# A chunked recurrence with two pairs of heads side by side: one row half per head, next inputs and last states in the gaps

## The reference

```python
for t in range(S):
    cur = einsum('bhd,bhe->bhde', u * k[t], v[t])
    y[t] = einsum('bhd,bhde->bhe', r[t], state + cur)
    state = w[t][..., None] * state + einsum('bhd,bhe->bhde', k[t], v[t])
```

## Time and profile before

| | us |
|---|---|
| median of 3 runs | 654.47 (654.16 to 656.38) |
| span of the profiled execution (first to last instruction) | 648.8 |
| of it: up to the first level of round 0 | 20.4 |
| round 0 | 28.3 |
| rounds 1 to 7 | 291.9 |
| last states, outputs, transposes of X | 21.1 |
| mixture up to its last stage | 55.6 |
| last stage | 231.5 |

### The profile page before, as it was taken

The page is one execution under the profiler, slowest core; times in us unless marked ns, Lnnn a source line. Parts: engine busy times, 40 slices in busy tenths (PEclk is TensorE's granted clock), DMA queues, the critical chain, the costliest instruction groups (busy, mean ns, idle before and its releaser), DMA issues.

```text
span 648.8 us, 20419 instructions
## 1 busy us (share of the span) xinstructions
PE 519.0 (80%) x8010; PEld 445.8 (69%) x8010; DVE 436.0 (67%) x968; ACT 397.5 (61%) x753; POOL 64.7 (10%) x79
## 2 busy tenths in 40 slices
PE   3756766877668668766686798699999999999996
PEld 2544655756457447564576434399999999999996
DVE  5668999898688688896797441465555555555553
ACT  3648686885576477865765313466566666656563
POOL 4011213112031031130310000000000000000000
PEclk9869898987698699886887899899999999999999
DMA  9995354362154143630057699311010101101010
GB/s 140 303 314 98 62 96 68 73 109 54 24 109 78 30 83 76 108 60 17 3 113 257 225 387 364 141 52 37 2 37 1 38 1 36 37 0 36 1 37 36
DMA packets 143325, 60.75 MB, mean 94 GB/s; under 512 B 126496, under 2 KB 139808, under 8 KB 142880
## 3 DMA queue, kind: packets, MB, share of 16 engines
q1 hardware_dynamic: 141264, 51.97, 33.9%
q10 hardware_dynamic: 2000, 7.86, 3.2%
HBM read 55.10 MB, written 4.72 MB: 92 GB/s over the span
## 4 chain that ended last, share of the span: by engine, by line
PE 63%; issue 13%; DVE 11%; ACT 10%; ACTq 1%; DVEq 1%; DMA 0%; SPq 0%
PE bank L708 11%; PE bank L710 10%; PE bank L709 10%; PE lbank L497 7%; ACT rkw L756 6%; PE tbank L449 4%; PE ybank L523 4%; PE bank L698 3%; DVE wprod L992 3%; DVE a_pack L1046 2%; PE tbank L459 2%; DVE rkw L1012 2%; PE bank L647 2%; PE bank L624 2%; PE bank L561 1%
## 5 line engine op out<-in xcount | busy, mean ns | idle before, releaser
L708 PE MATMUL bank<-wo_high,h_high 128*128 128x384 f32 x384 | 129.6, 337 | 1.8 <-DVE h_low L1212 1.6
L709 PE MATMUL bank<-wo_low,h_high 128*128 128x384 f32 x384 | 128.9, 336 | 0.0
L710 PE MATMUL bank<-wo_high,h_low 128*128 128x384 f32 x384 | 128.9, 336 | 0.0
L497 PE MATMUL lbank<-rhat,rkw 128*32 128x64 f32 x3456 | 81.5, 244 | 53.9 <-DVE a_pack L1046 36.8
L791 ACT ACTIVATE rhat<-rkw 48x384 f32<-48x384 f32 x160 | 85.0, 531 | 59.5 <-PE lbank L497 42.2
L497 PEld LDWEIGHTS lbank<-rhat,rkw 128*32 128x32 f32 x3456 | 69.9, 126 | 63.7 <-issue 61.9
L1210 DVE CAST h_high<-h_sq 128x384 fp32r<-128x384 f32 x128 | 46.0, 360 | 96.7 <-PE bank L710 87.9
L907 ACT ACTIVATE h_relu<-bank 128x384 f32<-128x384 f32 x128 | 62.9, 492 | 74.4 <-PE bank L698 74.1
L756 ACT ACTIVATE rkw<-tbank 128x384 f32<-128x384 f32 x96 | 74.4, 876 | 20.5 <-PE tbank L449 20.5
L449 PE MATMUL tbank<-ident,nat 128*128 128x128 f32 x288 | 62.7, 358 | 29.7 <-ACT rkw L756 16.7
L708 PEld LDWEIGHTS bank<-wo_high,h_high 128*128 128x128 f32 x384 | 72.6, 189 | 3.2 <-issue 2.8
(11 more groups left out here) (129 smaller groups left out, 639.2 us busy)
## 6 DMA issues: line engine op xcount, KB each, us to landing
w_sb<-in_moe_w_dram ACTq DMA_DIRECT2D x5, 1536.0 KB, 15.7
w_hi<-in_moe_w_dram SPq DMA_DIRECT2D x16, 384.0 KB, 8.1
nat<-in_r_dram SPq DMA_DIRECT2D x32, 144.0 KB, 3.2
nat<-in_k_dram SPq DMA_DIRECT2D x32, 144.0 KB, 3.8
nat<-in_w_dram SPq DMA_DIRECT2D x32, 144.0 KB, 3.9
mov<-in_v_dram SPq DMA_DIRECT2D x32, 144.0 KB, 3.3
v_tok<-in_v_dram SPq DMA_DIRECT2D x32, 144.0 KB, 3.3
w_sb<-in_moe_w_dram SPq DMA_DIRECT2D x3, 1536.0 KB, 7.4
```

Source lines behind the costliest of these rows:

```text
L497: last = nc.tensor.matmul(dst.rearrange("p (h t) -> p h t", h=2), kk[:, t0:t0 + SUB], rhat[s][:, :, tt:tt + SUB], start=True, stop=True)
L708: nc.tensor.matmul(acc, hi, wo_high[:, fb, :], start=(fb == 0), stop=False)
L709: nc.tensor.matmul(acc, hi, wo_low[:, fb, :], start=False, stop=False)
L710: last = nc.tensor.matmul(acc, lo, wo_high[:, fb, :], start=False, stop=(fb == NF - 1))
```

## The change

Four things change in the recurrence, and a few small ones around it.

- **Row halves.** `rhat`, `stat` and `mov` are gone. In levels 0, 4 and 5 each head is multiplied alone, with its own 64 rows of the array (`src[a:b, ...]`), 64 (level 5: 96) stationary columns and 64 or 32 moving ones. Only levels 1, 2 and 3 (`WIDE`) still use a padded copy, `wide`, filled by `widen` on ScalarE with the two copies that `r_to_rhat` had. The matrix `aa` stays where it is merged and is used as stationary tile directly (`y_near`, 24 matmuls of 64 rows), the state product is a second set of matmuls into the same bank (`y_far`, 22, since chunk 0 has no state before it). GpSimd has only its clearing at the start left.
- **Joined updates.** r and k lie in one tile, so one DVE instruction of 768 elements does `r_update` and `k_update` (`update`). The products of w are made for both pairs at once, for the next round, in one run of six instructions (`w_pairs`). u is multiplied in as ScalarE copies the inputs out (a scale of the activation), which takes four more copies a round and drops `heads_tilde`. The merge of level 0 has 768 elements, those of levels 1 to 4 have 384. Each input copy writes every second element (`half::2`), since a DMA now brings tokens in pairs.
- **Order.** The transposes of the next round's inputs go between the levels, one to three at a time (`T_ORDER`), as do the products of the last round. There are three copies of `rk` and two of `aa` and `wl`, used in turn. All eight rounds are written out; no loop is left in the recurrence, and `keep_warm` is gone from it. In the last round half of the transposes of X take the place of the next inputs.
- **Loads.** Inputs come in 24 transfers of 72 KB a round instead of 12 of 144 KB, v in 4 instead of 8. Three experts' `w1` are loaded in quarters within rounds 0 to 2, three in the last round and two after it; before, five came in round 0 and three from the last round on.
- **Mixture.** `keep_busy` puts 25 matmuls of 128 columns on constants at seven waits of the mixture.

The core of the diff:

```diff
-            def k_update(rd, s, lv):
+            def w_pairs(rd):
+                for s in range(2):
+                    dve.wait_ge(t_evac, t_out[t_use[rd, s, 2, 1]])
+                    if rd > 1:
+                        dve.wait_ge(w_spread[s], rd - 1)
+                buf = wl[rd % 2]
+                for lv in range(LEVELS):
+                    if lv:
+                        dve.wait_ge(w_pair, 6 * rd + lv)
...
+            def update(rd, s, lv):
+                m = 1 << lv
+                if lv:
+                    dve.wait_ge(level_mm[s], 6 * rd + lv + 1)
+                    dve.wait_ge(updated[s], 6 * rd + lv)
+                    dve.wait_ge(w_pair, 6 * rd + lv)
+                else:
+                    dve.wait_ge(t_evac, t_out[t_use[rd, s, 1, 1]])
+                by = w_level(rd % 2, s, lv).rearrange("p (n two) -> p two n", two=2).unsqueeze(3)\
+                    .to_broadcast([112, 2, S // (2 * m), m])
+                nc.vector.tensor_tensor(scaled_half(rk[rd % 3][s], m), scaled_half(rk[rd % 3][s] if lv else rt[s], m), by,
+                                        ALU.mult).then_inc(updated[s], 1)
...
+            for rd in range(ROUNDS):
+                for s in range(2):
+                    merge(rd, s, 0)
+                for lv in range(1, 5):
+                    for s in range(2):
+                        update(rd, s, lv)
+                        merge(rd, s, lv)
+                        if lv == 4 and s == 0 and rd < ROUNDS - 1:
+                            w_pairs(rd + 1)
+                    if lv < 3 and rd > 0:
+                        scan(rd - 1, lv - 1)
+                for s in range(2):
+                    update(rd, s, 5)
+                    if rd < ROUNDS - 1:
+                        update(rd + 1, s, 0)
...
+            def input_out(rd, s, x, half):
...
+                with_u = half == x
+                evac(use, rt[s][0:112, x, half::2], src, 2 * rd + s if with_u else None)
+                if with_u:
+                    evac(use, rk[rd % 3][s][0:112, x, half::2], src)
...
+                if late:
+                    kv_out(rd - 1, 0)
+                widen(rd, 0, 2)
+                if late:
+                    kv_out(rd - 1, 1)
+                next_out(0, 1)
+                widen(rd, 1, 2)
+                next_out(1, 2)
+                widen(rd, 0, 3)
...
-            with pe.Fori(1, ROUNDS) as rd:
-                round_(rd, True)
...
+                level(rd, 0, 1)
+                if late:
+                    k_times_v(rd - 1, 0)
+                level(rd, 1, 1)
+                if late:
+                    k_times_v(rd - 1, 1)
+                next_inputs(rd, 0, 1)
+                level(rd, 0, 2)
+                next_inputs(rd, 1, 2)
+                level(rd, 1, 2)
+                next_inputs(rd, 3, 2)
+                level(rd, 0, 3)
+                if late:
+                    y_near(rd - 1, 0)
```

## The result

The changed kernel takes 526.76 us (median of four runs, 525.12 to 528.74); the kernel before, timed beside it, 654.32 (646.10 to 656.38). The ratio is 0.8105, with a 95% interval of 0.8035 to 0.8175. Some executions of a kernel run slower at a lower granted clock; ratios compare only the faster ones, so they are not quotients of the medians, which take all. The profiled execution took 525.12 us with a span of 523.3.

The account below looks back on a forecast made before the run. DVE was taken to bound an undisturbed old round, DVE and ACT together the new one. Start 18.5, round 0 21, rounds 1 to 7 182, tail 15, mixture 54, last stage 231.5 make 522, plus 5.7: 528 us, range 503 to 550.

Parts of the forecast that it names:

- outside the span: Whole kernel: the median of the runs lies 5.7 us above the profiled span, so 522 becomes 528.
- Sum 20.8 us: TensorE's work in a new round at full clock, 20.8 us; TensorE is not the bound while the clock is up.
- levels 1 to 3 are paced by ACT, the end of the round by DVE and ACT together: Inside a round: ACT's queue sets the early levels, DVE and ACT the end; 25 us a round before disturbances.
- 23.2 and 23.3: Work in a new round: DVE 23.2 us instead of 35.1, ACT 23.3 us instead of 28.7.
- all 12 updates would suffer if GpSimd still copied: DVE updates in a round: GpSimd's SBUF reads would delay them, as a product took 1.42 us against 0.54.
- The allowance of 1 us a round: Recurrence rounds: half of the former 8% for clock and issue disturbances, raising 25 to 26 us a round.
- Coupling (559 us): Rival: in the recurrence, engine queues couple more tightly than placed, 30 us a round instead of 26; chance 0.12.
- Slow copies (575 us): Rival: input copies with a step of two cost 0.88 us like those with six, 32.3 us a round; chance 0.07.
- Clock (584 to 640 us): Rival: at half clock TensorE's 20.8 us a round become about 40 in the recurrence; chance 0.07.
- Code (659 us): Rival: straight-line rounds expose 41 instruction transfers at 3.2 us each, 131 us, slower than before; chance 0.04.
- Tail and mixture: After the rounds: tail 15 us instead of 21.1; mixture 54 instead of 55.6, with a gain at the first softmax.
- The start's gain: Before round 0: 18.5 us instead of 20.4, from shorter input copies, while loads hold most of it.

Follow-up runs that it names:

- pe_plus: Changed kernel with 18 more constant matmuls on TensorE ahead of the levels in each of rounds 1 to 6; 541.79 us.
- dve_plus: Changed kernel with four more DVE reductions of 0.95 us, behind merges of pair 1, in each of rounds 1 to 6; 528.9 us.
- far_flat: Changed kernel with `y_far` reading its moving state tile contiguously instead of with a step of 48 bytes (wrong states multiplied); 522.94 us.
- pool_plus: Changed kernel with 20 GpSimd copies of 48x128 from SBUF to SBUF in each of rounds 1 to 6; 528.45 us.
- act_plus: Changed kernel with 12 more small ACT copies, three ahead of each widen of levels 2 and 3, in each of rounds 1 to 6; 545.19 us.
- wide_none: Changed kernel without any padded copy: levels 1, 2 and 3 also multiply each head alone; 560.95 us.
- before_unrolled: Kernel before with rounds 1 to 7 written out instead of a hardware loop, nothing else changed; 635.91 us.
- wide1_c: Changed kernel with only level 1 on the padded copy, levels 2 and 3 multiplying each head alone; 542.23 us.
- no_busy_c: Changed kernel without the 25 constant matmuls of the mixture; 531.19 us.

## Why the prediction came out right, and where it was not

The time was forecast within 1.3 us (528 against 526.76), in part by luck. One step, the engine that bounds a round, was wrong, and other terms made up for it. The 5.7 us "outside the span" were wrong too: in every timed execution whose span is on record, of both kernels, the time is 1.7 to 2.0 us above the span. The 5.7 came of comparing the median with the span of a profiled execution that was faster than it; that difference does not lie outside the first and the last instruction. The two executions at the median of the changed kernel have spans of 524.9 and 525.0, 3 us above the sum of 522, and the term outside is 3.9 too large, so the two cancel.

| term | predicted, us | measured in the profiled execution, us |
|---|---|---|
| start | 18.5 | 15.8 |
| round 0 | 21 | 22.4 |
| rounds 1 to 7 | 182 | 182.5 |
| tail | 15 | 17.9 |
| mixture | 54 | 55.5 |
| last stage | 231.5 | 229.1 |
| span | 522 | 523.3 |
| outside the span | 5.7 | 1.8 |

- **Which engine bounds a round: wrong.** "Sum 20.8 us. TensorE is not the bound while the clock is up" failed. TensorE has 24.3 us and is the fullest; `pe_plus` and `dve_plus` show that work added to it counts nearly whole and work added to DVE hardly. Of "levels 1 to 3 are paced by ACT, the end of the round by DVE and ACT together" the first half came true (ACT without a wait up to level 3), and in the second TensorE is full, 11.64 of 11.64 us. The mis-sized terms are the output products, 5.4 us instead of 3.4 (2 x 1.53 and 2 x 1.18, priced at 0.85 each after `k_times_v`), and the levels, 10.8 instead of 9.0 (ten at 0.83 to 0.86, two of 96 stationary columns at 1.17, priced at 0.75). A number of `k_times_v` was carried to products with 64 stationary columns, to a moving tile with a step, and to `y_near`. Of `y_far` the step is shown (0.35 us each). `y_near` takes 1.53 us for 24 matmuls where level 4 takes 0.83 for 24, and where `y_far` in `far_flat`, with the same 64 stationary and 48 moving columns, takes 0.83 for 22. In `y_near` each row half writes only to the column half of the same number, so two of the four 64x64 tiles are used instead of four. That this is the cause is argued from the code; it wasn't tried.
- **DVE and ACT: the sizes held.** 23.2 and 23.3 were called tops; 22.0 and 21.3 were measured. Updates 0.954 us, none near 1.4. That "all 12 updates would suffer if GpSimd still copied" did not come true for the short copies of `pool_plus`. Copies 0.53 (bounds 0.45 and 0.88), 0.61 with the scale by u. kv copies 0.44, predicted 0.55. The joined merge took 1.015, predicted 0.96. The two merges of level 1 (m = 2) were longer than their price of 0.579: 1.01 us each (124.89 above), where those of m = 4 to 16 take 0.55 to 0.60. It is hidden, as DVE has room.
- **The allowance of 1 us a round: right in size, wrong in kind.** It stood for disturbances of clock and issue. The clock stayed at 1.00, and outside rounds 2 and 3 hardly any issue gap stands; TensorE's extra 3.5 us and the 1.3 in which it waits for ACT filled that place. The 25 us of an undisturbed round were 25.6. That DVE's old share (0.91) of a sum of 23.3 gives 25.6 too is a coincidence. Round 2 has the disturbance that was meant (27.85 us), with two gaps of 0.90 and 0.92 us, at 69.88 and 81.32.
- **Coupling (559 us): the mechanism is there, the size isn't.** The rival had "copies of inputs ahead of a widen that is ready", and that is what stands at 124.84 to 126.00. `act_plus` shows that 3.7 us more put there lengthen a round by 3.1. In the changed kernel it costs TensorE two waits of 0.49 and 0.35 us a round, not 4 us.
- **Slow copies (575 us): no.** The Trainium skill (SBUF — State Buffer, on the 16-byte lines) has a step of two at full rate and a step of six not; 0.53 beside 0.878 us agrees.
- **Clock (584 to 640 us): no.** TensorE busy 24.3 of 25.6 us kept 1.00, where 27.3 of 38.6 had 0.91. The stretches at half clock in `wide_none` are what this rival described.
- **Code (659 us): a small piece of it.** No gap of 3 us came; the two of round 2 are 0.90 and 0.92. But straight-line code has gaps: 9.8 us in rounds 1 to 7 of `before_unrolled`, 15.1 between 15 and 200 us in `wide_none`, 12.5 in `wide1_c`. The Trainium skill (Runtime: NRT & Kernel Launch, instruction fetch) has straight code fetched ahead; that the branch's own waits go agrees with it, the gaps inside the rounds of these kernels don't. When code comes late is open: gaps stand where matmuls are densest a microsecond or where inputs and expert weights are under way, and no run held one of these fixed.
- **Tail and mixture.** The tail was 2.9 us longer than summed: the output products of a pair take 2.7 us there and not 1.6, 2.2 in all, and two issue gaps of 0.61 and 0.87 us stand in it. In the mixture the first part gained 2.6 us and the second lost 2.4. The sum had the gain at the softmax, and put at nothing what it leads to: a transfer of expert weights, whose wait stands in every trace with the constant matmuls and in none without.

```profile
283.66 1.50 PE L714 MATMUL bank<-w_hi,h_t 128*32 128x384 f32 x16 [1.55 <-DMA w_hi<-in_moe_w_dram]
```

- **Where the 125.5 us of span came from:** rounds 1 to 7 109.4, round 0 5.9, start 4.6, tail 3.2, mixture 0.1, last stage 2.4, whose code is unchanged but which no longer begins at half clock; 2.2 of it are due to the constant matmuls ahead of it (`no_busy_c`), a term that the sum put at nothing. Of the 109.4 us, 21.7 are what the seven rounds of before took above the 38.6 of round 2, the rest is 38.6 against 26.1. How that divides among row halves, joined updates and the new order is not shown: no run undoes one of them, only the loop was tried by itself. The start's gain was put at 1.9; its DMA share fell from 1.11 to 0.89, as less is loaded before round 0.

## What to carry to other kernels

Price a matmul group by one with the same stationary columns, the same step of the moving tile and the same use of the array's quarters; halves that run beside each other in one group need not do so in the next. When work is taken off one engine, add up all engines again with the same care: here the old bound shrank by a third, and the engine with the lowest of the three sums turned out the fullest. Room on an engine over a whole round says little about one stretch of it: ask where its queue has no gap, and what stands there ahead of the instruction that others wait for. When constant work keeps the clock up, look behind it as well: here what it won was lost again at the next transfer, and what the traces show as won stood a stage later.

## What the runs showed of the hardware

- 24 float32 matmuls on 64 rows each, with row halves and column halves crossed, take as long as 12 on 128 rows (0.83 and 0.85 us). 24 that use only two of the quarters took 1.53; that the quarters are the cause was not tried.
- A moving float32 tile of 48 columns with a step of 48 bytes costs 0.35 us more for 22 matmuls than a contiguous one (1.18 and 0.83, `far_flat`).
- A predicated copy of 384 elements whose runs are two long takes 1.01 us, with runs of four or more 0.55 to 0.60.
- A GpSimd copy in the SBUF that begins during a DVE product or scan lasts until 0.15 or 0.09 us behind its end (up to 1.11 us instead of 0.29, 45 times in `pool_plus`), and DVE is not delayed. A product that begins during a GpSimd copy of 1.2 us takes 1.42 us instead of 0.54.
- TensorE can stand on issue in straight-line code: up to 3.64 us at once in `before_unrolled`, and 12.5 and 15.1 us between 15 and 200 us in the two kernels with 48 and 72 more matmuls a round, against 2.4 in the changed one.
